# Loops written out, first stages reordered across VectorE and ScalarE, and zero products between TensorE's first groups

## The reference

```python
scores = scale * np.matmul(q, k.transpose(0, 1, 3, 2))
mask = (rel >= 0) & (rel < 64)            # rel = query position - key position
scores = np.where(mask, scores, -1e9); attn = np.exp(scores - max)
attn = attn / (sum + 1e-09)
x = np.matmul(attn, v)                    # then heads are put side by side: 2304 x 512
h = x @ w_in;  x = np.maximum(0.01 * h, h) @ w_out        # layer 1
h = x @ w_in2; out = (h * np.cos(h)) @ w_out2             # layer 2
```

## Time and profile before

| what | us |
|---|---|
| median of 3 runs (lowest, highest) | 900.41 (899.0, 901.78) |
| the profiled execution | 900.46 |
| its span, first to last instruction | 897.7 |
| TensorE busy in the span | 871.0 |
| VectorE, ScalarE, GpSimd busy | 418.1, 369.6, 90.3 |

### The profile page before, as it was taken

The page is one execution under the profiler, slowest core; times in us unless marked ns, Lnnn a source line. Parts: engine busy times, 40 slices in busy tenths (PEclk is TensorE's granted clock), DMA queues, the critical chain, the costliest instruction groups (busy, mean ns, idle before and its releaser), DMA issues.

```text
span 897.7 us, 13153 instructions
## 1 busy us (share of the span) xinstructions
PE 871.0 (97%) x5040; PEld 719.9 (80%) x5040; DVE 418.1 (47%) x751; ACT 369.6 (41%) x849; POOL 90.3 (10%) x72
## 2 busy tenths in 40 slices
PE   5889999999999999999999899999999999999998
PEld 4778877787778877788888688888888888888897
DVE  4466444435443444443223454454455445544554
ACT  5566434334334343433444433343334333433443
POOL 3565000000000000001444300000000000000000
PEclk9999999999999999999999999999999999999999
DMA  6466202111112111004332400020002000200010
GB/s 207 153 193 218 75 26 75 63 37 61 50 63 75 35 63 50 13 1 142 101 100 84 139 1 0 0 93 0 0 0 93 0 0 0 72 1 1 1 48 23
DMA packets 29838, 52.90 MB, mean 59 GB/s; under 512 B 2528, under 2 KB 5984, under 8 KB 29792
## 3 DMA queue, kind: packets, MB, share of 16 engines
q1 hardware_dynamic: 29792, 52.24, 18.1%
HBM read 42.80 MB, written 9.44 MB: 58 GB/s over the span
## 4 chain that ended last, share of the span: by engine, by line
PE 90%; ACT 4%; DVE 3%; issue 2%; DMA 0%; POOL 0%; SPq 0%; DVEq 0%; ACTq 0%
PE h_ps L348 42%; PE y_ps L373 21%; PE y_ps L367 21%; PE st_ps L299 2%; PE st_ps L282 2%; PE st_ps L288 1%; ACT probs L444 1%; ACT w_hi L432 1%; DVE probs L590 1%; DVE neg_max L597 1%; ACT probsT L452 1%; DMA qk_sb<-qk 0%; DVE g_raw L643 0%; ACT g_hi L490 0%; DVE g_lo L665 0%
## 5 line engine op out<-in xcount | busy, mean ns | idle before, releaser
L348 PE MATMUL h_ps<-x_hi,w_hi 128*128 128x512 f32 (+1 forms) x640 | 242.2, 378 | 4.8 <-DVE g_raw L659 3.0
L348 PE MATMUL h_ps<-x_lo,w_hi 128*128 128x512 f32 (+1 forms) x640 | 237.4, 371 | 0.0
L348 PE MATMUL h_ps<-x_hi,w_lo 128*128 128x512 f32 (+1 forms) x640 | 237.3, 371 | 0.0
L348 PEld LDWEIGHTS h_ps<-x_hi,w_hi 128*128 128x128 f32 x640 | 122.0, 191 | 28.9 <-DVE g_raw L659 3.4
L665 DVE TENSOR_TENSOR g_lo<-g_raw,g_hi 128x512 fp32r<-128x512 f32 (+1 forms) x160 | 105.1, 657 | 85.8 <-ACT g_hi L490 85.8
L348 PEld LDWEIGHTS h_ps<-x_lo,w_hi 128*128 128x128 f32 x640 | 122.0, 191 | 20.6
L348 PEld LDWEIGHTS h_ps<-x_hi,w_lo 128*128 128x128 f32 x640 | 122.0, 191 | 19.6
L490 ACT ACTIVATE g_hi<-g_raw 128x512 fp32r<-128x512 f32 (+1 forms) x160 | 94.2, 589 | 104.6 <-DVE g_raw L643 52.6
L643 DVE TENSOR_TENSOR g_raw<-h_ps,act_in 128x512 f32<-128x512 f32 (+1 forms) x80 | 51.0, 637 | 175.0 <-ACT act_in L469 175.0
L256 POOL TENSOR_TENSOR w_lo<-w_raw,w_hi 128x512 fp32r<-128x512 f32 x64 | 86.1, 1367 | 409.6 <-ACT w_hi L432 409.4
L367 PE MATMUL y_ps<-g_hi,w_hi 128*128 128x512 f32 (+1 forms) x320 | 121.2, 379 | 0.1
(11 more groups left out here) (53 smaller groups left out, 789.4 us busy)
## 6 DMA issues: line engine op xcount, KB each, us to landing
qk_sb<-qk SPq DMA_DIRECT2D x36, 288.0 KB, 3.1
v_sb<-values SPq DMA_DIRECT2D x36, 256.0 KB, 2.8
w_raw<-w_in SPq DMA_DIRECT2D x32, 256.0 KB, 2.7
w_raw<-w_out SPq DMA_DIRECT2D x32, 256.0 KB, 2.8
layer_out<-y_out SPq DMA_DIRECT2D x4, 1024.0 KB, 5.8
x_raw<-layer_out SPq DMA_DIRECT2D x4, 1024.0 KB, 7.5
out<-y_out SPq DMA_DIRECT2D x4, 1024.0 KB, 5.0
mask_sb<-mask SPq DMA_DIRECT2D x4, 256.0 KB, 3.0
```

Of the source, the lines that this page charges most:

```text
L348: mm = pe.matmul(h_ps[:, j % 2, 0:width], w[:, j, cols], x[:, kt, 0:width], start=kt == 0 and a == 0, stop=kt == KT - 1 and a == 2)
```

## The change

ScalarE's and VectorE's and TensorE's loops become Python loops, so that all chunks are written out. Weight halves come in the order of the table `ORDER`: w_in two tiles ahead of w_out in layer 1. The first four halves are rounded by VectorE. At the start GpSimd scales pairs 0 and 1, VectorE pairs 2 and 3; x is split straight from PSUM instead of from a copy in `x_raw`; TensorE makes nine products of a zeroed tile between its first groups. In `attention`, transposes and their copy move to slot 4 of the step, the copy ahead of the exponentials, and VectorE's `row_max` ahead of `copy_o`.

```diff
+ORDER = ([(t, 0) for t in range(LEAD)] + [(t + d, half) for t in range(FT - LEAD) for d, half in ((LEAD, 0), (0, 1))]
+         + [(t, 1) for t in range(FT - LEAD, FT)] + [(t, half) for t in range(FT, 2 * FT) for half in range(2)])
+ON_DVE = 4
...
# SP
-            sp.dma_start(ident_sb[:], ident).then_inc(ident_in, 16)
             load_qk(2)
             load_qk(3)
+            sp.dma_start(ident_sb[:], ident).then_inc(ident_in, 16)
             load_v(0)
             load_weights(0)
             load_v(1)
             load_weights(1)
+            load_v(2)
             load_weights(2)
-            load_v(2)
+            load_v(3)
             load_weights(3)
-            load_v(3)
...
# GpSimd
+                if u < ON_DVE:
+                    pool.wait_ge(w_hi_first, u + 1)
+                else:
+                    pool.wait_ge(w_hi_done, u - ON_DVE + 1)
...
+            for p in range(2):
                 pool.wait_ge(inv_done, p + 1)
...
+                pool.tensor_tensor(rows, rows, inverse, ALU.mult).then_inc(pool_probs_done, 1)
+            for u in range(4 * FT):
                 split_half(u)
...
# TensorE
-                if r == 7 and 1 <= p < PAIRS:
+                if r == 4 and 1 <= p < PAIRS:
                     transposes(c, p - 1)
...
+            def idle(count, st):
+
+                for _ in range(count):
+                    pe.matmul(st[:, 0, 0:PAIR], act_in[:, 0, 0:P], act_in[:, 0, 0:PAIR], start=True, stop=True)
...
+            pe.wait_ge(zero_in, 1)
+            idle(3, st_ps)
+            first_scores(0)
+            idle(2, st_ps)
+            first_scores(1)
+            idle(1, st_ps)
+            first_scores(2)
+            idle(1, st_ps)
+            first_scores(3)
+            pe.wait_ge(ident_in, 16)
+            pe.wait_ge(scores_read, 1)
+            idle(1, first_banks[0])
+            first_transposes(0)
+            idle(1, first_banks[0])
+            first_values(0)
+            first_transposes(1)
+            first_transposes(2)
+            first_values(1)
+            first_transposes(3)
+            first_values(2)
+            first_up(0)
+            first_values(3)
+            for kt in range(1, KT):
+                first_up(kt)
...
-            with nc.Fori(N1, LAST - 1, engines=(pe.engine,), hint_back_edge=True) as n:
+            for n in range(N1, LAST):
                 chunk(n, 2, False)
-            chunk(LAST - 1, 2, False)
...
# ScalarE
-                if r == 2 and p < PAIRS:
+                if r == 4 and 1 <= p < PAIRS:
+                    copy_transposed(c, p - 1, st_ps)
+                if r == 4 and p < PAIRS:
                     exps(c, p)
-                if r == 8 and 1 <= p < PAIRS:
-                    copy_transposed(c, p - 1, st_ps)
...
                     if is_first(n) and j + EARLY < FT:
-                        split_weights(j + EARLY)
+                        split_half(2 * (j + EARLY))
+                        split_half(2 * (j + EARLY) + 1)
...
             def first_x_block(kt):
-                act.wait_ge(o_copied, kt + 1)
-                split_x_block(kt, FIRST)
+                act.wait_ge(pv_done, kt + 1)
+                act.activation(x_hi[:, kt, 0:FIRST], first_banks[kt][:, 0, PAIR:2 * PAIR], ACT.Copy).then_inc(x_hi_done, 1)
...
             exps(0, 2)
-            split_half(0)
+            exps(0, 3)
             copy_transposed(0, 1, first_banks[1])
-            exps(0, 3)
-            split_half(1)
             first_x_block(0)
             copy_transposed(0, 2, first_banks[2])
-            split_half(2)
+            copy_transposed(0, 3, first_banks[3])
             first_x_block(1)
             first_x_block(2)
-            copy_transposed(0, 3, first_banks[3])
-            split_half(3)
             first_x_block(3)
...
-            with nc.Fori(1, N1 - 1, engines=(act.engine,), hint_back_edge=True) as n:
+            for n in range(N1 - 1):
                 chunk(n, 1, True)
...
# VectorE
                 if r == 1 and p < PAIRS:
                     scale_mask(c, p, st_ps)
+                    row_max(c, p)
                 if r == 1 and 2 <= p <= PAIRS:
                     copy_o(c, p - 2, st_ps)
-                if r == 1 and p < PAIRS:
-                    row_max(c, p)
...
+            def split_half(u):
+                t, half = ORDER[u]
+                dve.wait_ge(w_raw_in[u], 16)
+                dve.tensor_copy(w_hi[:, t, half * DM:half * DM + DM], w_raw[:, u, :]).then_inc(w_hi_first, 1)
...
+            dve.memset(act_in[:, 0, 0:PAIR], 0.0).then_inc(zero_in, 1)
+            first_mask(0)
+            first_mask(1)
+            invert(0, 0)
+            first_mask(2)
+            invert(0, 1)
+            first_mask(3)
+            split_half(0)
+            split_half(1)
+            invert(0, 2)
+            normalise(0, 2)
+            invert(0, 3)
+            normalise(0, 3)
+            first_x_block(0)
+            split_half(2)
+            first_x_block(1)
+            split_half(3)
+            first_x_block(2)
+            first_x_block(3)
...
-            with nc.Fori(N1, LAST - 1, engines=(dve.engine,), hint_back_edge=True) as n:
+            for n in range(N1, LAST):
                 chunk(n, 2, False)
```

More of the change, by code:

```diff
@@ L179, in load_weights @@
                     sp.wait_ge(w_ready, u - WSTAGES + 1)
[L180 to L181 removed]
+                t, half = ORDER[u]
+                src = (w_in, w_out)[half]
+                sp.dma_start(w_raw[:, u % WSTAGES, :], src[t]).then_inc(w_raw_in[u % WSTAGES], 16)
             def load_x(n):
@@ L261, in normalise_first @@
                 inverse = bass.AP(tensor=row_inv, offset=4 * p, ap=[[4 * PRING, P], [1, 4], [0, P]])
-                pool.tensor_tensor(rows, rows, inverse, ALU.mult).then_inc(probs_done, 1)
-            normalise_first(0)
-            normalise_first(1)
-            split_half(0)
-            normalise_first(2)
-            split_half(1)
-            normalise_first(3)
-            for u in range(2, 4 * FT):
+                pool.tensor_tensor(rows, rows, inverse, ALU.mult).then_inc(pool_probs_done, 1)
+            for u in range(4 * FT):
                 split_half(u)
@@ L342, in up_part @@
                     pe.wait_ge(x_hi_done, KT * n + kt + 1)
+                if is_first(n) and j < LEAD and kt == 0:
+                    pe.wait_ge(x_ready, 1)
                 width = width_of(n, layer)
@@ L411, in _, with first_up @@
                 value_tiles(p, first_banks[p])
-                for kt in ([], [], [0], [1, 2, 3])[p]:
-                    for j in range(LEAD):
-                        if kt == 0:
-                            weights(1, j, 0)
-                        up_part(0, j, kt, 1)
+            def first_up(kt):
+                for j in range(LEAD):
+                    if kt == 0:
+                        weights(1, j, 0)
+                    up_part(0, j, kt, 1)
+            pe.wait_ge(zero_in, 1)
[22 more added lines that the diff above has]
+                first_up(kt)
             for n in range(N1 - 1):
@@ L573, in _ @@
             split_weights(2 * FT - 1)
-            with nc.Fori(N1, LAST - 1, engines=(act.engine,), hint_back_edge=True) as n:
+            for n in range(N1, LAST):
                 chunk(n, 2, False)
-            chunk(LAST - 1, 2, False)
             chunk(LAST, 2, False, last=True)
@@ L614, in copy_o @@
             def copy_o(c, p, st):
-                hp, t0 = (p, 0) if is_first(c) else (p // 2, PAIR * (p % 2))
+                hp, t0 = p // 2, PAIR * (p % 2)
                 dve.wait_ge(pv_done, pair(c, p) + 1)
-                if p == 0 and not is_first(c):
+                if p == 0:
                     dve.wait_ge(x_ready, KT * c)
@@ L709, in chunk, with first_mask, first_x_block @@
                                 hidden_lo(m, i, ahead)
-            for p in range(PAIRS0):
+            def split_half(u):
+                t, half = ORDER[u]
+                dve.wait_ge(w_raw_in[u], 16)
+                dve.tensor_copy(w_hi[:, t, half * DM:half * DM + DM], w_raw[:, u, :]).then_inc(w_hi_first, 1)
+            def first_mask(p):
                 scale_mask(0, p, first_banks[p])
                 row_max(0, p)
-                if p >= 1:
-                    invert(0, p - 1)
-            for p in range(PAIRS0):
-                copy_o(0, p, first_banks[p])
-                split_x_block(0, p, FIRST)
-                if p == 0:
-                    invert(0, PAIRS0 - 1)
+            def first_x_block(kt):
+                dve.wait_ge(x_hi_done, kt + 1)
+                dve.tensor_tensor(x_lo[:, kt, 0:FIRST], first_banks[kt][:, 0, PAIR:2 * PAIR],
+                                  x_hi[:, kt, 0:FIRST].bitcast(F32), ALU.subtract).then_inc(x_ready, 1)
+            dve.memset(act_in[:, 0, 0:PAIR], 0.0).then_inc(zero_in, 1)
[17 more added lines that the diff above has]
+            first_x_block(3)
             for j in range(LEAD):
@@ L723, in _ @@
                 hidden_lo(0, j, 1)
```

(6 more changed lines are left out.)

43 lines of the change are left out of this document (24 added, 19 removed).

## The result

The changed kernel takes 886.39 us (median of 4 runs, 885.21 to 887.74), the kernel before 900.99 in the runs beside it (899.0 to 901.78): a ratio of 0.985, 95% interval 0.983 to 0.986. The forecast was 883.9 with a range of 876 to 893. The profiled execution took 886.43, its span 884.6.

| stretch | before | after | saved | forecast |
|---|---|---|---|---|
| to the scores of chunk 0 | 28.30 | 23.40 | 4.9 | 6.1 |
| from there to layer 2's first down products (503.16; 494.90) | 474.86 | 471.50 | 3.4 | 5.55 |
| from there to its last six (892.79; 879.54) | 389.63 | 384.64 | 5.0 | 4.9 |
| behind it, and outside the span | 7.7 | 6.9 | 0.8 | 0 |

A forecast was written before the change was run, and what follows sets the result against it. TensorE was taken as the bound, losing time only in the start, chunk 0 and the entry of the second loops. Savings of 6.1 + 5.55 + 4.9 = 16.55 us from 900.46 give 883.9 us, range 876 to 893.

The forecast's parts named there:

- The loops: Entry of chunk 5: written-out code removes VectorE's 6.99 us idle time at the branch, saving 4.9 us, ends 0 and 4.9.
- Rival B: Entry of chunk 5: the wait stays because two 1 MB transfers fill the queues; 888.8 us, chance 0.13.
- The start: Before chunk 0: a shorter chain through all engines ends at 22.2 instead of 28.3 us, saving 6.1, ends 3.8 and 8.4.
- Zero products: Start: each of nine taken at 0.85 us, half if they lift the clock; both cases lie between the start's ends.
- Chunk 0: First chunk: 7.3 + 0.6 + 1.7 - 0.3 - 3.75 = 5.55 us saved, ends 1.2 and 10.1.
- The first term: Chunk 0: with transposes and their copy earlier, all 7.3 us of values waiting for probsT go.
- The transposes' new waits: Chunk 0: transposes wait 1.25 us for VectorE's mask operation in three of four rounds, 3.75 us, ends 0 and 5.8.
- The qk wait: Chunk 0: scores still wait for pair 5's qk load, 1.4 to 1.7 us, so 0.3 worse.
- the 1.7 us of the clock: Chunk 0: with shorter pauses the clock's fall between 80 and 88 us goes, giving 1.7 us back.
- A: Nothing is late next: no wait in the transposes' place and an early fast clock; 878.0 us, chance 0.24.
- C: The start gains little and the first chunk inherits late weights: 3.8 + 1.2 + 4.9 saved, 890.6 us, chance 0.13.
- D: Slower: VectorE's first execution of straight code waits 4.9 us at chunk edges 2, 3, 6, 7; 903.5 or 908.4 us, chance 0.03.

The follow-up runs named there:

- e1: The kernel before with all five loops written out and nothing else changed: 894.81 us, ratio 0.994 to the kernel before.
- e2: The changed kernel with VectorE's second loop (chunks 5 to 7) put back: 886.18 us, ratio 0.984 to the kernel before.
- e9: The changed kernel with only VectorE's first loop (chunks 1 to 3) put back: 886.12 us, ratio 0.984 to the kernel before.
- e6: The changed kernel with both loops of VectorE put back (chunks 1 to 3 and 5 to 7): 891.14 us, ratio 0.991 to the kernel before.
- e10: The changed kernel with VectorE's inverse and scaling at slot 5 and five more zero products in the start's pause: 883.41 us, ratio 0.981 to the kernel before.
- e5: The changed kernel with VectorE's inverse and scaling at slot 5 of a step instead of slot 8: 884.55 us, ratio 0.983 to the kernel before.
- e3: The changed kernel without its nine zero products: 886.41 us, ratio 0.984 to the kernel before.
- e8: The changed kernel with the attention steps in the old order in all chunks: 890.41 us, ratio 0.989 to the kernel before.
- e4: The changed kernel with the qk loads of pairs 5 to 11 two steps earlier in SyncE's queue: 888.64 us, ratio 0.986 to the kernel before.
- e12: The changed kernel with scaling at slot 5, qk two steps ahead, five more zero products, chunk 0's first mask operation and maximum earlier: 879.97 us, ratio 0.977.
- e11: The changed kernel with VectorE's scaling at slot 5 and qk loaded two steps ahead: 884.43 us, ratio 0.983 to the kernel before.
- e7: The changed kernel with all five loops of all engines put back: 890.37 us, ratio 0.990 to the kernel before.

## Why the prediction was right, and where its terms were not

**The loops: right, 4.9 forecast and 5.0 in the trace** (5.4 in e1's medians). The reason given for it, a branch into the loop, was half of it. The Trainium skill (Runtime: NRT & Kernel Launch, Instruction fetch mechanics) says that a taken branch beyond the fetched code stalls; e2 and e9 each take a branch into a loop at no cost that shows, and only the two in one list bring 6.93 us. If the rule is to fit, the code must have been fetched already in e2 and not in e6, and no run shows what was fetched. Rival B (the two 1 MB transfers) is out: the transfers are issued in every build, and only builds with both loops stall.

**The start: 4.9 instead of 6.1, within its ends.** The step that was mis-sized is the middle between "everything at its shortest" and "at its longest". Of what stands between the exponentials and the last up product, VectorE's scaling of pair 2 was near its longest (1.50 of 1.63) and the first operation of its inverse, which takes 0.17 alone, took 0.89 (the sum has 0.4 for the whole inverse), both beside GpSimd, and they made the pause of 2.94 us behind which four groups took 0.74 to 1.12 instead of 0.66. e10 bears out this second part: with five zero products in the pause the groups take 0.66 to 0.69, chunk 0 begins 0.66 us earlier than in e5 and the median is 1.1 us lower, though the intervals of the two ratios overlap.

**Zero products: the price was right** (0.85 taken at the slow level, about 0.95 measured for each of the first three; 0.43 at the fast, 2.32 / 5 = 0.46 measured), and their gain was put within the ends. The nine gain nothing that e3 can tell: they raise the clock early, and it falls again behind the pause.

**Chunk 0: 3.4 instead of 5.55.** The first term, 7.3 us for the order of attention, held as a wait that goes: the waits for probsT are gone, and e8, with the old order, has 4.6 us of them again. With the new wait of 3.75 taken off, the forecast has 3.55 for the order, and e8 measures 3.25 (trace) to 4.0 (medians). So did the 0.6 us of w_lo. Three others were off. The transposes' new waits were put at 3 x 1.25 = 3.75 us and measured 0.40, 0.35 and 1.02: too high by 2.0, because a late qk delays scores and leaves VectorE time to catch up, which the count of one round left out; e4, with no qk wait, has 3.63, 1.14, 1.15 and 1.14, so the count's 1.25 was near for the rounds that it describes. (Its terms, 5.4 + 3.7 + 0.4 + 0.7, give 10.2 and a wait of 1.35, not 10.1 and 1.25; without the meeting with GpSimd they leave 0.4 a round, 1.2 in all, not 0.5; and the 0.9 in the chunk's worst end has no source.) The qk wait was put 0.3 us worse and is 2.98 + 0.66 + 0.71 = 4.35 in place of 1.4: 2.95 worse. That the load "starts earlier by as much as the chunk does" held to 0.01 us; what failed was to take its landing as unchanged. It took 1.6 us longer, and the cause stays open. The DMA engines were 83% busy in the window before it (24 to 28 us) against 40% (28 to 32) in the kernel before, but e1 speaks against that as the reason: there they were 29% busy ahead of the load (30 to 33 us) and it took 4.82 us all the same. While it was under way they were busier in the kernel before (88%) than in the changed one (81%). The changed order is not needed for the long wait either, since e1 has it with the old order: the 1.4 that the sum started from was the shorter of the two traces of that chunk 0. In the other builds that have this load at its place the stretch from issue to scores is 3.65 (e6) to 4.58 us (e9). The other 1.37 us are two later pairs whose scores the shorter chunk now reaches before their loads have landed. And the 1.7 us of the clock did not come back: it fell elsewhere, behind the 2.98 us of the first qk wait. In sum 7.3 + 0.6 + 0.2 (a wait of the transposes for the mask operation, 0.23 at 39.73 us before, which the forecast left out) - 1.8 - 2.95 = 3.35, the 3.4 of the trace.

So part of the closeness is luck: 2.0 us too much for the transposes stand against 2.65 too little for qk and 1.7 for the clock. By the prediction's own sign of being wrong, a pause beyond those it lists, its picture of the pauses failed in part: it has one wait for qk where there are three, and no wait of 2.94 us in the start.

The errors in the two waits are bound together: the waits for qk and for the mask operation stand in parallel, and each hides the other. e4 removes one and gains nothing, e5 removes the other and gains 1.8 (medians), and both, with the first pair's mask operation ahead and the pause filled, give e12's 6.4.

**The rivals.** A (nothing late next) fell: something was late. Its 878.0 is near e12's 879.97, a kernel with four more edits. C (start and chunk at their worst) was right that both would fall short of the middle, but neither came to its end. D is refuted: VectorE's longer straight list has no wait of its own.

## What to carry to other kernels

When a wait is taken off an engine, the next one is seldom alone: read all semaphores that the waiting instruction needs, since a late transfer can hide a late VectorE, and removing either by itself shows nothing (e4) or a part (e5). Keep VectorE's two-input operations out of the time of GpSimd's where TensorE waits for them; three slots earlier was enough here. Fill a pause of TensorE with zero products where the work behind it is on the path (e10), not where it will pause again. And don't carry a wait for a load from one trace into a sum as if it were fixed: the same chunk had 1.4 us of it in one trace and 3.1 in another.

## What the runs showed of the hardware

A pause of TensorE is followed by the 1.2 GHz level only sometimes. In chunk 0, pauses of 2.98 (changed kernel) and 2.64 us (e5) were followed by windows of 0.79, and one of 2.40 us (e10) by slow products at once (1.13 us for the scores); one of 2.15 (e2), one of 2.64 (e11) and one of 2.88 us (e9) were not, so the length of the pause alone does not decide it. e9's:

```profile
32.45 0.67 PE L286 MATMUL st_ps<-qk_sb 64*64 64x128 f32 x16 [2.88 <-DMA qk_sb<-qk]
```

```profile
32.00:40.00 8.00, 6.84 (x88) 6.21 (x88) 6.64 (x12) 5.21 (x17) 5.69 (x4) 1.00 0.66 210
```

So a loss of 1.7 us comes and goes between builds of nearly equal work, which no sum over waits can place. It comes and goes between executions of one kernel too: the four of the changed kernel have mean clocks of 0.997, 0.994, 0.995 and 0.992 and take 885.21, 886.36, 886.43 and 887.74 us.

VectorE's 6.9 us at a loop's entry came only with an earlier loop in the same engine's list (the kernel before, e6, e7), with the same operations between them. A loop alone, early (e9) or late (e2), cost nothing that five executions could tell.
